# k of later head pairs turned by VectorE in 32x32 blocks instead of by TensorE, in a fused attention and mixture-of-experts kernel

## The reference

```python
q_bits = (einsum('bhsd,dk->bhsk', q, proj) > 0); k_bits = (einsum(..., k, proj) > 0)
mask = q_bucket[..., :, None] == k_bucket[..., None, :]      # all 6 bits equal
scores = where(mask, scale * q @ k.T, -1e9)
attn = softmax(scores)                                       # over the row
x = attn @ v            # B=2, H=8, S=768, D=64
x = moe(x)              # 8 experts, the best two for each token
x = rational(x @ w_in) @ w_out
```

## Time and profile before

| what | value |
|---|---|
| median of three runs | 1000.24 us |
| profiled execution, its own time | 1002.7 us |
| its span, first to last instruction | 1001.1 us |
| PE, PEld busy over the span | 93%, 80% |
| DVE, ACT, POOL busy over the span | 59%, 50%, 40% |
| attention (pair 0 begins at 16.4 us, PE's last values matmul starts at 303.9 us) | about 290 us of the span |
| mean granted TensorE clock | 0.974 of full |

### The profile page before, as it was taken

How to read it: one execution, slowest core, us unless ns; L and a number is a source line. 1 busy time by engine, 2 the same in 40 slices (tenths; PEclk the granted TensorE clock), 3 DMA queues, 4 the chain that set the end, 5 groups by cost and what they waited for, 6 DMA issues and landing times.

```text
span 1001.1 us, 17998 instructions
## 1 busy us (share of the span) xinstructions
PE 935.4 (93%) x5673; PEld 805.0 (80%) x5674; DVE 592.9 (59%) x1257; ACT 500.7 (50%) x914; POOL 402.9 (40%) x344
## 2 busy tenths in 40 slices
PE   6999999999991899999999999998489999999998
PEld 5788888888871688888888888887379999999997
DVE  6888888888876223222222232221299877878775
ACT  3677777777660222222222222221277777777775
POOL 4401120110243446645563635520577655463222
PEclk9999999999996899999999999999599999999999
DMA  9762423323133867778886768733621110110000
GB/s 203 208 178 55 99 49 81 71 52 87 43 117 128 272 204 246 258 235 246 266 266 207 250 186 275 258 122 105 199 82 50 38 54 22 52 34 9 33 1 31
DMA packets 115476, 134.45 MB, mean 134 GB/s; under 512 B 57186, under 2 KB 75106, under 8 KB 114914
## 3 DMA queue, kind: packets, MB, share of 16 engines
q1 hardware_dynamic: 73778, 63.01, 21.7%
q0 software_dynamic: 19328, 54.53, 17.1%
q10 hardware_dynamic: 22320, 16.26, 5.6%
HBM read 114.12 MB, written 19.66 MB: 134 GB/s over the span
## 4 chain that ended last, share of the span: by engine, by line
PE 81%; DVE 9%; ACT 3%; issue 3%; DMA 1%; POOL 1%; ACTq 0%; another core or an unknown queue 0%; SPq 0%; DVEq 0%; POOLq 0%
PE ps_s L1068 17%; PE ps_o L1093 17%; PE ps_s L1136 13%; PE ps_t L1122 6%; PE ps_t L947 4%; PE ps_o L960 4%; PE ps_s L1122 4%; PE ps_m L1122 3%; PE ps_s L1079 3%; PE ps_s L938 3%; DVE mx L1216 2%; PE ps_s L939 2%; PE ps_m L913 2%; DVE den L1228 1%; PE ps_o L972 1%
## 5 line engine op out<-in xcount | busy, mean ns | idle before, releaser
L534 POOL TENSOR_TENSOR w_r<-raw,w_r 128x1024 f32 (+1 forms) x72 | 171.9, 2403 | 111.9 <-DMA raw<-in_moe_w 48.9
L1068 PE MATMUL ps_s<-w_r,xT 128*128 x744 | 179.6, 398 | 17.0 <-DVE xT L1428 17.0
L1093 PE MATMUL ps_o<-w_r,hT 128*128 x744 | 175.6, 392 | 2.6 <-DVE hT L1432 2.6
L1068 PEld LDWEIGHTS ps_s<-w_r,xT 128*128 128x128 f32 x744 | 139.2, 190 | 45.3 <-issue 17.3
L1093 PEld LDWEIGHTS ps_o<-w_r,hT 128*128 128x128 f32 x744 | 140.8, 189 | 32.1 <-issue 2.8
L1136 PE MATMUL ps_s<-w_r,g_r 128*128 128x512 f32 x576 | 144.0, 395 | 3.8 <-DVE g_r L1514 3.8
L1438 DVE COPY y_sb<-ps_o 128x512 f32<-128x512 f32 x31 | 21.4, 691 | 211.6 <-PE ps_o L1093 211.6
L1136 PEld LDWEIGHTS ps_s<-w_r,g_r 128*128 128x128 f32 x576 | 106.6, 188 | 24.0 <-issue 3.7
L793 ACT ACTIVATE hT<-ps_s 128x1024 fp32r<-128x1024 f32 x31 | 31.8, 1027 | 160.2 <-DVE y_sb L1438 105.8
L654 POOL TENSOR_TENSOR m<-q,g_r 128x384 f32<-128x384 f32 x64 | 65.9, 1030 | 113.2 <-DVE g_r L1502 113.0
L713 ACT ACTIVATE prob<-ps_s,nb,sc 128x768 f32<-128x768 f32 x96 | 95.2, 992 | 23.3 <-DVE nb L1221 22.5
(11 more groups left out here) (241 smaller groups left out, 1504.7 us busy)
## 6 DMA issues: line engine op xcount, KB each, us to landing
w_r<-in_moe_w POOLq DMA_DIRECT2D x32, 1024.0 KB, 8.5
raw<-in_moe_w SPq DMA_DIRECT2D x56, 512.0 KB, 4.0
xg<-x_slots ACTq DMA_DIRECT2D x124, 64.0 KB, 3.1
y_slots<-y_sb ACTq DMA_DIRECT2D x31, 256.0 KB, 4.5
q_in<-in_q SPq DMA_DIRECT2D x16, 384.0 KB, 4.3
k_in<-in_k SPq DMA_DIRECT2D x16, 384.0 KB, 5.2
raw<-in_moe_w SPq DMA_DIRECT2D x16, 256.0 KB, 4.3
raw<-in_moe_w_in SPq DMA_DIRECT2D x8, 512.0 KB, 5.8
```

What stands on the lines that cost most here:

```text
L534: pool.tensor_tensor(of_chunk(buf, 1, n), raw[:, par, :], of_chunk(buf, 0, n).bitcast(F), ALU.subtract).then_inc(split_done, 1)
L1068: mm = pe.matmul(ps_s[0][:, o * 512:o * 512 + 512], xT[:, par, part, c * P:c * P + P], w_r[:, buf, wpart, col:col + 512], start=(c == 0 an ...
L1093: mm = pe.matmul(ps_o[:, :], hT[:, part, c * P:c * P + P], w_r[:, buf, wpart, col:col + DM], start=(c == 0 and part == 0 and wpart == 0), ...
```

## The change

Five things change.

1. k of pairs 1 to 7 no longer goes through PE. SP loads a head of k in four DMAs (`load_tile`), one for each 32 partitions, so laid out that 32x32 blocks turned in place give the whole transpose. DVE turns all 24 blocks of a head in one instruction into `tile_t` (`turn_tile`), ACT rounds the 768 columns in one instruction (`round_tile`), and POOL writes the remainder into `km` (in `copies`). Pair 0 is prepared as before.
2. The points have new tables: turns of q and all bits are laid out anew over the steps (`PE_AT`, `DVE_AT`), the turn of the tile is at points (0, 2) and (3, 2), written (step, point), its rounding at (1, 1) and (4, 1), and the bits of k at steps 2 and 5.
3. The bits of k wait on PE for POOL's remainder (`tile_split`).
4. `tile_t` takes the place of part of the second raw buffer, so the eighths of expert 0 come through one buffer, each loaded after the one before it is used, and `refill` has a new order.
5. `rs` and `den` hold the row sums of the two heads apart ([P, 2, T] for [P, T, 2]).

The core of the diff:

```diff
-    POINTS = [(kind, i) for i in range(len(PREP)) for kind in ("turn", "bits")]
...
+    PE_AT = {(0, 0): ("turn", 0), (0, 1): ("bits", 0), (1, 0): ("turn", 1), (1, 1): ("bits", 1), (2, 0): ("bits", 2), (2, 2): ("bits", 3),
...
+    TURN_AT = {(0, 2): 0, (3, 2): 1}
+    ROUND_AT = {(1, 1): 0, (4, 1): 1}
...
+            def load_tile(m, hh):
+                rows = head_rows(k, m, hh).rearrange("(a i) (t d) -> i a t d", a=Q, d=D)
+                run = T * D - P // Q
+                for g in range(Q):
+                    part = slice(g * (P // Q), (g + 1) * (P // Q))
+                    src = rows.rearrange("i a t d -> i a (t d)")[:, :, g % 2 * (P // Q):g % 2 * (P // Q) + run]
+                    sp.dma_start(k_quad[part, :, 0:run], src).then_inc(tile_loaded, 16)
...
+                sp.wait_ge(tile_turned, n * 2 + 1)
+                load_tile(n + 1, 1)
                 if qk:
...
+                    sp.wait_ge(chunk_turned, q_chunk(n + 1, 1))
+                    load_rows(n + 2, 0, q_in, q, q_loaded["qA"])
+                sp.wait_ge(split_done, n + 1)
+                load_first_raw(n + 1)
...
             def copies(n, half, par, first, last):
...
+                first_split(n)
                 if last:
                     return
+                for hh in range(2):
+                    copy_q(n + 1, 1 - par, 4 * hh)
+                    copy_q(n + 1, 1 - par, 4 * hh + 1)
+                    pool.wait_ge(tile_hi, n * 2 + hh + 1)
+                    pool.tensor_tensor(km[0:64, 1 - par, hh, :], tile_t[0:64, :], kh[0:64, 1 - par, hh, :].bitcast(F),
+                                       ALU.subtract).then_inc(tile_split, 1)
...
-            for loaded in qk_loaded.values():
+            for loaded in q_loaded.values():
                 pool.wait_ge(loaded, 16)
+            pool.wait_ge(tile_loaded, 16 * Q)
...
+            def round_tile(n, mpar, hh):
+                act.wait_ge(tile_turned, n * 2 + hh + 1)
+                act.activation(kh[:, mpar, hh, :], tile_t[:], ACT.Copy).then_inc(tile_hi, 1)
...
             def bits(m, mpar, i):
-                pe.wait_ge(chunk_split, m * NP + i + 1)
+                if w == "q" or isinstance(m, int) and m == 0:
+                    pe.wait_ge(chunk_split, q_chunk(m, i))
+                else:
+                    pe.wait_ge(tile_split, (m - 1) * 2 + (hh + 1))
+                    pe.wait_ge(chunk_done, m * NP + i)
...
+            def turn_tile(n, hh):
+                dve.wait_ge(tile_loaded, (n * 2 + hh) * (16 * Q) + 16 * Q)
+                if not (isinstance(n, int) and n * 2 + hh == 0):
+                    dve.wait_ge(tile_split, n * 2 + hh)
+                dve.transpose(tile_t[:].rearrange("p (t a j) -> p t a j", t=T, a=Q),
+                              k_quad[:].rearrange("p a (t d) -> p t a d", d=D)[:, :, :, 0:P // Q]).then_inc(tile_turned, 1)
...
-                dve.tensor_scalar(den[:, t, :], rs[:, t, :], 1e-9, None, ALU.add).then_inc(den_done, 1)
+                dve.tensor_scalar(den[:, :, t], rs[:, :, t], 1e-9, None, ALU.add).then_inc(den_done, 1)
```

More of the change, by code:

```diff
@@ L104, in fused_kernel @@
     nb = small("nb", [P, 4], F)
[L105 to L106 removed]
+    rs = small("rs", [P, 2, T], F)
+    den = small("den", [P, 2, T], F)
     rinv = small("rinv", [P, T, 2], F)
@@ L547, in expert_halves, with first_split @@
                         (w2[bass.ds(e, 1)].rearrange("a (c p) d -> (a p) c d", p=P), DM))
-            def first_split(n, par):
-                pool.wait_ge(raw_loaded[par], n // 2 * 32 + 32)
-                pool.tensor_tensor(of_first_chunk(1, n), raw[:, par, :].rearrange("p (s n) -> p s n", s=2),
-                                   of_first_chunk(0, n).bitcast(F), ALU.subtract).then_inc(split_done, 1)
-            def copies(n, half, par, first, last):
[L557 to L561, removed]
+            def first_split(n):
+                if isinstance(n, int) and n == 0:
+                    for part in range(4):
+                        pool.wait_ge(hi_loaded[part], 16)
+                pool.wait_ge(first_loaded, n * 32 + 32)
+                pool.tensor_tensor(of_first_chunk(1, n), raw[:, 0, :].rearrange("p (s n) -> p s n", s=2),
+                                   of_first_chunk(0, n).bitcast(F), ALU.subtract).then_inc(split_done, 1)
@@ L571, in _ @@
-            copies(-1, -1, 1, True, False)
+                for hh in range(2):
[4 more added lines that the diff above has]
+                                       ALU.subtract).then_inc(tile_split, 1)
+            for i in (0, 1, 4, 5):
+                copy_q(0, 0, i)
@@ L996, in point @@
                     return
-                for kind, i in points(t, pt):
-                    if kind == "turn":
-                        turn(n + 1, i)
-                    else:
-                        bits(n + 1, 1 - par, i)
+                kind, i = PE_AT.get((t, pt), ("", 0))
+                if kind == "turn":
+                    turn(n + 1, i)
+                elif kind == "bits":
+                    bits(n + 1, 1 - par, i)
             def steps(n, half, par, first, last):
@@ L1329, in point @@
                     return
-                for kind, i in points(t, pt):
-                    (split if kind == "turn" else bits)(n + 1, 1 - par, i)
+                kind, i = DVE_AT.get((t, pt), ("", 0))
+                if kind == "turn":
+                    split(n + 1, 1 - par, i)
+                elif kind == "bits":
+                    bits(n + 1, 1 - par, i)
+                if (t, pt) in TURN_AT:
+                    turn_tile(n, TURN_AT[t, pt])
             def steps(n, half, par, first, last):
```

88 lines of the change are left out of this document (50 added, 38 removed).

## The result

The changed kernel takes 1021.58 us in the median (1020.53 to 1022.95), 21.3 us more than the 1000.24 us given for before. Beside runs of the kernel before on the same chip (median 999.79) the ratio is 1.0225, with a 95% interval of 1.0208 to 1.0243. So the direction was as forecast, and the size was not: 1007.2 us had been predicted, and the time lies above the range of 998.5 to 1014.0. The profiled execution took 1022.5 us with a span of 1020.9 us, where before had 1001.1.

The account below looks back on a forecast made before the run. PE and DVE were taken as nearly full, taking turns as the bound of a 34.8 us pair. 13.5 us lost in pair 0 less 6.5 gained later gave 7.0 more: 1000.24 to 1007.2 us, range 998.5 to 1014.0.

Parts of the forecast that it names:

- The stall: Pair 0: PE waits from about 30 to 43.8 us for POOL's k remainder, queued behind `first_split`; 13.5 us lost in all.
- the casts land at 38.0: Start of pair 0: the four casts `first_split` waits for land at 38.0 us, range 36.5 to 41.5, before at 41.50.
- The rest of pair 0: Pair 0 after the stall: 21.3 us of steps plus 2.3 us for a lower clock, so pair 1 begins at 67.4.
- The gain of 1.2 us a pair: Pairs 1 to 5: each 1.2 us shorter, bounds 0 and 2.9, so 6.0 us in all.
- the two floors: A pair's least time by engine after the change: PE 32.9 us, DVE 31.9 us, for 34.8 before.
- Pair 6: The pair with routing work also on DVE, 38.3 us and bound by DVE: 0.5 us gained.
- The third, POOL in DVE's way: Rival: DVE's small sum waits for POOL 1 to 1.8 us more a pair, gain gone, 1013.7 us; chance 0.20 with no gain.
- The first, the whole slack: Rival: pairs fall to 31.9 us, or 32.9 at worst; 15.5 us gained against 13.5 lost, 998.2 us; chance 0.13.
- The second, no stall: Rival: pair 0 does not stall, `first_split`'s wait being over by 35 us; only the gain is left, 993.7 us; chance 0.05.
- The transpose: DVE, two a pair of 128x768: 0.99 us each, between 544 ns and 1.43 us; would not wait for POOL.
- POOL's remainder: POOL, two k remainders of 64x768 a pair: 1.84 us each, bounds 1.02 and 2.39.
- the row layout: Row sums of the two heads laid out apart: costed at nothing, range 1.2 us less a pair to nothing.

Follow-up runs that it names:

- e7: The changed kernel with SP's loads of k B and q A for later pairs held until the four casts landed: 1021.19 us, ratio 1.0179.
- e1: The changed kernel with POOL's `first_split` of pair 0 moved behind that pair's copies of q and remainders of k: 1003.14 us, ratio 1.0036.
- e10: e9 with 13 of 14 DVE transposes turning only 128 of 768 columns (stale k, for time only): 978.1 us, ratio 0.9806.
- e4: The changed kernel without the addition of 1e-9 to the two row sums; the reciprocal reads the sums: 1015.57 us, ratio 1.0158.
- e5: The kernel before the change, without the addition of 1e-9 to the row sums: 995.46 us, ratio 0.9927.
- e6: The changed kernel with the edits of e1, e2 and e4 together: 999.35 us, ratio 0.9966.
- e9: e6 with PE's bits of q also one point later, at point 2, behind the values matmuls: 983.32 us, ratio 0.9856.
- e8: The changed kernel with the row sums of the two heads side by side again ([P, T, 2]): 1025.27 us, ratio 1.0221.
- e12: e5 run again on the chip of e9: 994.08 us, ratio 0.9954.
- e2: The changed kernel with q's places on DVE and ACT one point later, the remainder behind A's row maximum: 1018.05 us, ratio 1.0195.

## Why the prediction was right in direction and wrong in size

Up to pair 7, where the prediction had 7.0 us more, the profile has 23.3: 7.4 of the 16.3 us between them lie in pair 0, 9.6 in pairs 1 to 5, and 0.7 the other way in pair 6.

**The stall: right in place and releaser, mis-sized.** PE was to go on at 43.8 us and went on at 49.72. Of these 5.9 us, 6.0 are the term "the casts land at 38.0" (44.00 measured); the rest of that step, 5.8 us of POOL work, was right (5.7). It had three parts, and each was too favourable.

The largest is a load that was left out. SP's timeline of the kernel after:

```profile
24.15 1.75 SPq L430 DMA_DIRECT2D k_in<-in_k  x4
```

The k tile of head B is issued at 24.15, as soon as DVE has turned head A, and so right ahead of the casts; the lines of `refill` in the diff say so. The prediction had counted q alone beside the casts. The queues of after, 24 to 44 us (packets, MB, share of 16 engines, as in the earlier trace rows):

```profile
q0 software_dynamic: 1600, 4.19, 63.4%
q1 hardware_dynamic: 2128, 1.11, 30.5%
```

The second queue took 30.5% of 20 us of 16 engines, 97.6 engine-us. From 33.7 to 43.7 us it has q alone in it (1436 packets, nearly all of 256 B):

```profile
q1 hardware_dynamic: 1436, 0.36, 25.8%
```

That is 28.7 ns a packet (25.8% of 10 us of 16 engines over 1436), more than the 22.6 of the earlier trace rows. So the 1536 of q are 44.1 of the 97.6 engine-us, and the other 592, of which 512 are the tile's, 53.5: some 90 ns each, where the prediction had estimated 71. In e7, where neither tile nor q lie beside the casts, these land at 38.88 us, 5.1 us sooner. Shared out by engine-us, an estimate that no run tests, the tile has 2.8 of the 5.1 us and q 2.3.

Second, the constants came 0.3 us sooner (22.78 for 23.07) and not 1.5, so 1.2 us more. The queue ahead of them, 0 to 28 us (for the earlier trace rows):

```profile
q1 hardware_dynamic: 12875, 4.94, 87.3%
```

It has fewer packets, but they take 30.4 ns each (0.873 x 28 x 16 over 12875) and not 24.8, so it is no less busy. The third part is what remains of the 6.0, 2.0 us. Alone, the casts took 38.88 - 24.64 = 14.2 us from issue to use; before they took 41.50 - 24.78 = 16.7 us beside 3043 packets, whose share was 4.3 us. Taking those away gave 2.5 us and not 4.3. So a packet's share can't be subtracted whole from the time of the transfers beside it. e1 shows the whole stall on its own.

**The rest of pair 0: near.** 74.66 - 49.72 = 24.9 us where 23.6 were taken. The clock stayed at its lower level for some 5 us, as forecast from the earlier trace rows; steps of 6 us instead of 5.6 are the rest.

**The gain of 1.2 us a pair: wrong in sign.** This is the step that failed in kind. It took the two floors, 32.9 and 31.9 us, and gave the pair about two thirds of the slack of the engines. PE's floor was 0.9 us too high: e10 has 32.0. The step it was summed from, 5.93 us, held some 0.14 us of waits by the same sum (32.0 less four turns and eight bits leaves 4.42 us a step, not 4.56), and so the sum for before came to 34.6 and seemed to say that PE was full. With 32.0 + 1.7 = 33.7 us for the old k, it was not. More than that, neither floor sets the pace after the change. What does, from step 0 to 1 and from 3 to 4, is a loop over DVE, ACT and DVE again, 6.23 us round, in which the length of single instructions and waits counts and a turn of k on PE does not. What held a pair at 34.6 us before, without the sum, was not followed. The new tables put all four turns of q at a step's start, with DVE's remainder ahead of the A maximum; that lengthened the pair by 0.57 us (e4 against e5, and e6 takes it back) while the work taken from PE bought nothing. The prediction had said "Two engines take turns at being the bound", and that sentence should have led to following one loop through the new order. That the gain was there to be had is shown by e9: 32.5 us a pair, once both loops are open.

**Pair 6 and the end: small.** 1.2 us gained for the 0.5 forecast. (The prediction's 38.3 us for this pair was a stretch from 231.70 us; from A scores to A scores it took 37.60.) Of the 3.2 us behind it, 2.5 are not the change's.

**The rivals.** The third, POOL in DVE's way, foresaw that the gain would be gone and gave 1013.7 us. The wait it named exists and grew, from 1.22 to 1.67 us in one place, but 0.15 us of a pair's 0.72 are its share (e4, e5); the order has the rest. No rival named it: it had stood in the first only as a condition, "if the order of the points now fits both engines". The first, the whole slack, is what e9 reaches in the pairs, 32.5 us against its 31.9 to 32.9. The second, no stall, is refuted by the 19.76 us.

**The edits costed by themselves.** The transpose (0.978 us for 0.99), POOL's remainder (1.81 for 1.84) and the row layout at nothing (e8) were right. The Trainium skill's "Vector Engine (DVE) Microarchitecture Reference", section 5.1, had been read in the prediction as saying that the layout would not change the wait and that the transpose would not wait at all. e8 agrees with the first (1.68 us in either layout). On the second the runs say little: the transposes take 967 to 981 ns in all 14, but only the first of them lies beside instructions of POOL. In e4 it begins at 22.77 us, inside one that runs from 22.60 to 22.89, and takes 970 ns, which agrees.

**Open.** What makes the end of attention some 2.5 us longer in some profiles is not known; all four from the chip of e5 to e8 have it. The 0.7 us that is left of the 3.2, and the 1 us or so of e10's 5 us that lies outside the pairs, have no cause shown. They are no more than profiles of one kernel differ by in the stages behind attention: from the last matmuls with v to the end of the span e5 takes 695.0 us and e12 697.5.

## What to carry to other kernels

The sum of each engine's work bounds a stage from below, and says nothing of its pace until one loop has been followed through the new order, instruction by instruction, from one row maximum to the next. When an operation that feeds a busy engine moves to an idle one, the first thing to read is what stands ahead of it in the idle engine's queue, and which waits that holds: here one call, moved behind the copies and remainders of the first pair, was worth 1.9%. And freed work pays only when every loop is open: e2 and e6 opened one and found the next, e9 opened both and took 3.3 us off a pair of the changed kernel, 0.65 of them by leaving out the sum.

## What the runs showed of the hardware that was not expected

- A sum over two elements on DVE can wait through two POOL instructions in a row: 3.00 us in pairs 0 to 3 of e2, ended by the second. It need not: in pairs 4 and 5 it took 0.69 and 0.65 us and ended with the first, though the second followed at once. The Trainium skill, "SBUF — State Buffer", section "SBUF: two separate sides", says that the loser is blocked for the whole instruction of the winner; two in a row it does not tell of.
- A reciprocal of the same two elements never waited: 169 ns at most, with 7 of 48 wholly inside a POOL instruction in e4 and 12 in e9. Leaving the sum out gave 6.0 us (e4) and 0.5 to 0.7% (e5, e12).
- A packet of 1408 B into 32 partitions took some 90 ns of a DMA engine beside the casts, by the sum above, about three times the 28.7 ns of a packet of 256 B in the same stretch, for 5.5 times the bytes.
